# Attention inputs in smaller transfers: keys and queries in two pieces, values in four, each waiting for the piece four places ahead

## What is computed

```python
# q, k, v: (2, 8, 768, 64); tokens 2*768 = 1536, features 8*64 = 512
k_sum = k.reshape(B, H, 24, 32, D).max(axis=3)      # one maximum per block of 32 keys
v_sum = v.reshape(B, H, 24, 32, D).mean(axis=3)
scores_l = scale * q @ k.T, kept where |i - j| < 16  # banded
scores_s = scale * q @ k_sum.T + log(32)
a = softmax over [scores_l, scores_s];  attn = a @ [v, v_sum]
x = attn as (1536, 512)
x = relu(x @ w_in) ** 2 @ w_out                      # d_ff = 2048
h = x @ w_in2;  g = P(h) / Q(h);  out = g @ w_out2   # P cubic, Q of |h| and h*h
```

## Time and profile before

| what | value |
|---|---|
| median of three runs | 594.11 us (592.52 to 595.53) |
| the profiled execution's own time | 595.49 us |
| its span | 593.6 us |
| granted TensorE clock | full speed in all slices |
| matmul busy | 584.5 us, 98% |
| VectorE, ScalarE, GpSimd busy | 409.4, 290.6, 154.8 us |
| moved by DMA | 31.42 MB, most of it in the first 75 us and in the stretches in which weights are loaded |
| attention | 0 to about 72 us |

### The profile page before, as it was taken

One profiled execution on the slowest core, in us unless ns is written; L12 is line 12 of the kernel. 1 busy time (PEld: TensorE's weight loads), 2 busy tenths in 40 slices (PEclk: granted clock), 3 DMA queues, 4 the chain that ended last, 5 costly groups with the idle time before them and its releaser, 6 DMA issues.

```text
span 593.6 us, 10634 instructions
## 1 busy us (share of the span) xinstructions
PE 584.5 (98%) x3770; PEld 478.9 (81%) x3770; DVE 409.4 (69%) x791; ACT 290.6 (49%) x613; POOL 154.8 (26%) x159
## 2 busy tenths in 40 slices
PE   8999999999999999999999999999999999999997
PEld 5777788888888888888888888888888888888885
DVE  5888797663433233456666788888888888888885
ACT  5989511101301110311011887777777777867775
POOL 3768920000300000400000354353342212222221
PEclk9999999999999999999999999999999999999999
DMA  7886470000000000033223200000100000100001
GB/s 243 229 251 181 150 272 0 1 0 1 1 0 0 0 0 0 0 108 106 80 97 107 71 1 1 0 0 1 71 0 0 0 0 0 72 0 1 0 1 71
DMA packets 11618, 31.42 MB, mean 53 GB/s; under 512 B 1600, under 2 KB 2112, under 8 KB 11584
## 3 DMA queue, kind: packets, MB, share of 16 engines
q1 hardware_dynamic: 11296, 30.68, 15.9%
q10 hardware_dynamic: 288, 0.26, 0.1%
HBM read 27.79 MB, written 3.15 MB: 52 GB/s over the span
## 4 chain that ended last, share of the span: by engine, by line
PE 96%; ACT 2%; issue 1%; DVE 1%; POOL 0%; DVEq 0%
PE bank L565 44%; PE bank L633 22%; PE bank L650 22%; PE bank L551 2%; PE bank L535 2%; PE bank L501 1%; ACT prob L715 1%; PE bank L521 1%; PE bank L510 1%; PE bank L590 1%; PE bank L528 0%; DVE prob L934 0%; POOL prob L385 0%; DVE ksum L919 0%; DVE hlo L1079 0%
## 5 line engine op out<-in xcount | busy, mean ns | idle before, releaser
L565 PE MATMUL bank<-xhi,whi 128*128 (+1 forms) x384 | 149.9, 390 | 0.0
L565 PE MATMUL bank<-xhi,wlo 128*128 (+1 forms) x384 | 149.4, 389 | 0.0
L565 PE MATMUL bank<-xlo,whi 128*128 (+1 forms) x384 | 149.4, 389 | 0.0
L732 ACT ACTIVATE hsq<-bank 128x512 f32<-128x512 f32 x48 | 28.8, 600 | 213.2 <-PE bank L565 213.1
L443 POOL TENSOR_TENSOR denom<-denom,habs 128x512 f32<-128x512 f32 (+1 forms) x49 | 66.0, 1348 | 246.1 <-ACT denom L820 246.1
L565 PEld LDWEIGHTS bank<-xhi,wlo 128*128 128x128 f32 x384 | 72.1, 188 | 15.0
L565 PEld LDWEIGHTS bank<-xhi,whi 128*128 128x128 f32 x384 | 72.1, 188 | 14.9
L565 PEld LDWEIGHTS bank<-xlo,whi 128*128 128x128 f32 x384 | 72.0, 188 | 14.8
L650 PE MATMUL bank<-whi,hhi 128*128 128x512 f32 x192 | 75.0, 390 | 0.6 <-DVE hlo L1079 0.6
L1079 DVE TENSOR_TENSOR hlo<-ratio,hhi 128x512 fp32r<-128x512 f32 (+1 forms) x49 | 51.1, 1042 | 34.7 <-ACT hhi L803 34.6
L650 PE MATMUL bank<-wlo,hhi 128*128 128x512 f32 x192 | 74.7, 389 | 0.0
(11 more groups left out here) (80 smaller groups left out, 888.1 us busy)
## 6 DMA issues: line engine op xcount, KB each, us to landing
wraw<-w SPq DMA_DIRECT2D x29, 512.0 KB, 3.4
vwin<-vw SPq DMA_DIRECT2D x16, 288.0 KB, 4.0
out<-osb SPq DMA_DIRECT2D x12, 256.0 KB, 2.1
kraw<-kT SPq DMA_DIRECT2D x7, 384.0 KB, 4.9
q<-qT SPq DMA_DIRECT2D x7, 384.0 KB, 5.0
wraw<-w SPq DMA_DIRECT2D x6, 256.0 KB, 5.0
kraw<-kT SPq DMA_DIRECT2D x2, 128.0 KB, 2.8
q<-qT SPq DMA_DIRECT2D x1, 256.0 KB, 3.7
```

Of the source, the lines that this page charges most:

```text
L565: last = mm(hps[j % 2][:, :], W[a][:, j, kt * P:(kt + 1) * P], X[b][:, kt, bass.ds(CH * c, CH)], start=kt == 0 and i == 0, stop=kt == KT - ...
L732: a.activation(hsq[:, i, :], hps[i][:, :], ACT.Relu).then_inc(h_free, 1)
```

## The change

Keys and queries of a pair-batch n of 1 and more go in two transfers each (768 columns as 2 by 384, 192 KB each), values in four (12 windows as 4 by 3, 144 KB each, for n = 0 too). Each piece has a semaphore of its own. Before it is issued, each piece waits for the landing of the piece four places ahead in the order k, k, q, q, v, v, v, v: keys i for values i of n - 1, queries i for values 2 + i of n - 1, values i for keys i or queries i - 2 of n. The waits that protect buffers stay. TensorE and VectorE wait for each semaphore in turn at the places where they waited for one.

```diff
-    q_in = [sem(f"q_in{r}") for r in range(RING)]
+    q_in = [[sem(f"q_in{r}_{i}") for i in range(2)] for r in range(RING)]
-    k_in = [sem(f"k_in{r}") for r in range(RING)]
-    vw_in = [sem(f"vw_in{r}") for r in range(V_RING)]
+    k_in = [[sem(f"k_in{r}_{i}") for i in range(2)] for r in range(RING)]
+    vw_in = [[sem(f"vw_in{r}_{i}") for i in range(4)] for r in range(V_RING)]
...
         def load_k(n):
             if n >= RING:
                 sp.wait_ge(s_done, GPB * (n - RING + 1) + 1)
-            if n == 1:
-                sp.wait_ge(q_first[0], 16)
-            else:
-                sp.wait_ge(*q_landed(n - 1))
-            sp.dma_start(kraw[n % RING][:, BAND:BAND + S], kT[n]).then_inc(k_in[n % RING], 16)
+            for i in range(2):
+                sp.wait_ge(*vwin_landed(n - 1, i))
+                sp.dma_start(kraw[n % RING][:, BAND + S // 2 * i:BAND + S // 2 * (i + 1)],
+                             kT[n][:, S // 2 * i:S // 2 * (i + 1)]).then_inc(k_in[n % RING][i], 16)
...
         def load_q(n):
             if n >= RING:
                 sp.wait_ge(s_done, GPB * (n - RING + 1) + 2)
-            sp.dma_start(q[n % RING][:, :], qT[n]).then_inc(q_in[n % RING], 16)
+            for i in range(2):
+                sp.wait_ge(*vwin_landed(n - 1, 2 + i))
+                sp.dma_start(q[n % RING][:, S // 2 * i:S // 2 * (i + 1)],
+                             qT[n][:, S // 2 * i:S // 2 * (i + 1)]).then_inc(q_in[n % RING][i], 16)
...
-            if n > 0:
-                sp.wait_ge(*vwin_landed(n - 1))
-            for i, half in enumerate((slice(0, NW // 2), slice(NW // 2, NW))):
-                if n > 0 and i == 1:
-                    sp.wait_ge(*k_landed(n))
-                sp.dma_start(vwin[n % V_RING][0:KW, half, :], vw[n][:, half, :]).then_inc(vw_in[n % V_RING], 16)
+            for i in range(4):
+                if n > 0:
+                    sp.wait_ge(*(q_landed(n, i - 2) if i >= 2 else k_landed(n, i)))
+                part = slice(NW // 4 * i, NW // 4 * (i + 1))
+                sp.dma_start(vwin[n % V_RING][0:KW, part, :], vw[n][:, part, :]).then_inc(vw_in[n % V_RING][i], 16)
...
                 if n > 0:
-                    pe.wait_ge(q_in[r], 16 * (n // RING + (r > 0)))
+                    for i in range(2):
+                        pe.wait_ge(*q_landed(n, i))
...
-                    pe.wait_ge(k_in[r], 16 * (n // RING + (r > 0)))
+                    for i in range(2):
+                        pe.wait_ge(*k_landed(n, i))
...
-            pe.wait_ge(vw_in[n % V_RING], 32 * (n // V_RING + 1))
+            for i in range(4):
+                pe.wait_ge(*vwin_landed(n, i))
...
-                dve.wait_ge(k_in[r], 16 * (n // RING + (r > 0)))
+                for i in range(2):
+                    dve.wait_ge(*k_landed(n, i))
```

More of the change, by code:

```diff
@@ L236, in landing, with k_landed, q_landed, vwin_landed @@
         return (index - EARLY) % LAND, k + (index - EARLY) // LAND
[L238 to L248, removed]
+    def k_landed(n, i):
+        return k_in[n % RING][i], 16 * (n // RING + (n % RING > 0))
+    def q_landed(n, i):
+        return q_in[n % RING][i], 16 * (n // RING + (n % RING > 0))
+    def vwin_landed(n, i):
+        return vw_in[n % V_RING][i], 16 * (n // V_RING + 1)
     block = nc.Block()
```

## The result

The changed kernel takes 597.88 us (median of five runs, 597.36 to 598.08) against 595.26 us for the kernel before (median of five, 592.52 to 596.98). The ratio is 1.0061, with a 95% interval of 1.0041 to 1.0081: slower by 0.6%, some 3.6 us. The two medians alone lie 2.6 us apart, close to the lower end of that interval. The profiled execution has a span of 595.8 us, 2.2 us above the one of before; but that one lay 1.4 us above the median of the first three runs. So the two traces, read against each other, can account for 2.2 to 2.3 us and not for 3.6.

A forecast was written before the change was run, and what follows sets the result against it. TensorE was taken as the bound, its matmuls covering 584.5 of 593.6 us. Waits 0, issues 0 and landings 0 summed to 0, applied to the median of 594.11 us: 594.0 us, range 591.5 to 597.0.

The forecast's parts named there:

- T: Loads at the loop's start: time from a piece's issue to landing with four pieces under way, taken as 2.7 us.
- the one chain into which it was put: Values 0 to keys 3, one T per landing: keys 3 in at 20.2 us, inside 1.8 us of slack, cost 0.
- The straight line through the three sizes: Upper estimate of landing time from 128, 288 and 384 KB transfers: 2.9 us at 144 KB, 3.3 at 192, 3.1 average.
- The test of the pace: Load rounds in the attention: 2T = 5.4 us against the 7.0 us TensorE needs, so loads stay ahead.
- Rival B: Landings at the start slower than before, keys 3 stall TensorE before scores(8): 595.1 us at T = 3.1; chance 0.20.
- its second sign: Sign toward slower landings: a DMA by name among TensorE's waits, the alternative to a VectorE wait near 22 us.
- B's formula: TensorE loses time before scores(8) once keys 3, in at 3.97 + 6T, pass 19.77 + 1.8 us.
- The waits on TensorE: 38 more satisfied waits in scores and summaries: cost 0, upper bound 0.4 us.
- The 30 more issues on SyncE: 12 us more work on SyncE, hidden in its waiting time: cost 0, or 0.8 us once if uncovered.
- Rival A: TensorE's "issue" stalls (1.1 and 1.2 us, no visible cause) before 75 us vanish: 591.8 us, at best 590.9; chance 0.13.
- Rival C: 38 new instructions shift TensorE's code cuts; a 1.1 us stall comes or goes: 593.0 to 595.2 us; chance 0.12.

The follow-up runs named there:

- The count of places: The change with each piece waiting for the one three, five, six or eight places ahead, not four: 1.0195, 1.0020, 1.0009, 1.0006 against the kernel before.
- the kernel with the gap filled: The changed kernel plus seven 128-column matmuls where TensorE had waited 1.78 us for queries of pair-batch 2: 1.0070 against the kernel before, 599.4 us.
- the 38 waits: The kernel before with its loads untouched and 38 more satisfied waits on TensorE: 1.0010, 594.37 us beside 594.35.
- the bare stop: The kernel before, with TensorE also waiting for the keys of pair-batch 3 ahead of the scores of group 6: 1.0048, 597.69 us.
- the late start with six: The change with the first four pieces of pair-batch 1 held back as before, later ones waiting six places ahead: 0.9997 against the kernel before, 594.07 us.
- keys and queries 1 freed: The change, but keys and queries of pair-batch 1 do not wait for values of 0: 1.0072 against the kernel before, 598.52 us.

## Why the prediction was wrong, point by point

**Where the time is.** Right: nothing after 75 us moved, and the first feed-forward matmul came 2.30 us later. I had said under 1 us. Keys 1 were issued at 6.18 us, near the 6.3 forecast; VectorE's wait for keys 4 shrank from 0.82 to 0.45 us (now called "issue") and did not go. Wrong: that loads can only act where TensorE stands still. Of the 2.3 us, 1.6 us is busy time, nearly all of it (1.47 us) matmuls at the lower clock behind the stop.

**The step that failed is T, the time to landing, and the one chain into which it was put.** I took T = 2.7 us from a row of 128 KB at the start. Measured were 3.2, 2.9 and 3.9 us for values, keys and queries, weighted by their 32, 14 and 14 pieces 3.3 us. The straight line through the three sizes, which I had as the upper bound, gave 3.1 us and was nearer. I argued it down because less would be queued. The count of places shows how far that holds: with three places, values landed in 2.5 us, but keys and queries still took 3.3. The estimate of 2.4 us from the Trainium skill ("DMA: Bandwidth & Descriptors", "Anatomy of one DMA") was lower still; that section is on transfers issued by GpSimd, these are issued by SyncE, and the trace's 3.3 us decides.

The chain was wrong too. I followed only the keys, over VectorE. The chain that ended last runs through the queries: from the values issued at 4.30 us to the landing of queries 2 at 19.92 us it has four landings of 3.32 + 4.41 + 2.09 + 5.38 = 15.2 us, 3.8 us each, where my T gives 10.8. The scores of group 6 wait for these queries directly. At T = 2.7 they would have landed at 15.1 us and had 2.8 us to spare against 17.87; even at the mean of 3.3 they would have been in time, at 17.5. It took the long landings of single pieces, which no mean shows: the two halves of queries 2 took 5.5 us in the median. They also held back the keys of pair-batch 3. These were issued at 20.34 us, behind the last quarter of values 2, which had to wait for queries 2, and SyncE runs its program in order. That (23.75 - 3.97)/6 = 3.30 us agrees with the mean is therefore partly luck.

**The test of the pace was too weak.** I compared 2T with the 7.0 us that TensorE needs, found it smaller, and held the loads safe. With 4 pieces of 168 KB, 0.69 MB, under way and T = 3.3 us the rate is 209 GB/s, as the profile shows (207 from 14 to 28 us). A round then takes 6.6 us, and with the waiting between landing and issue 6.9 on average, single rounds 6.1 to 7.8: against 7.0 us that holds the pace but makes up little. Loads have to be faster than their user to win the lead that the start lacks.

**Rival B had the cause right, and the path wrong.** I gave it 0.20. Its threshold, T = 2.93, was passed, and its second sign came, a DMA by name among TensorE's waits. But TensorE never stopped for its path, keys 3 to block maxima to `masked(6)`: the scores of group 8 start at 26.38 us back to back with the work before them, as the stop for queries 2 and the slow stretch had already made TensorE later than keys 3 would have. (In the kernel with the gap filled these scores begin 25.61 - 24.33 = 1.28 us behind the block maxima; 23.75 + 1.28 = 25.0 us here, an estimate.) By B's formula T = 3.3 costs 3.97 + 19.8 - 21.57 = 2.2 us. That this is also the difference of the spans is luck: what made it up is the late keys of pair-batch 6, issued 6.3 us later than before where keys 3 had been 4.4 us late, less the "issue" stops of before that are gone. B's own path shows where the stop is filled with matmuls: the scores of group 8 then wait 0.59 us for VectorE, and with two whole transfers under way 1.55 us.

**The waits on TensorE**, 0 with 0.4 as a bound: nothing against it, though 1.0010 has an interval that is too wide (up to 2 us) to bear out a bound of 0.4 us. **The 30 more issues on SyncE**: with the waits of before, split transfers cost 0.14%, 0.8 us, where I had 0. What of that is issuing and what shorter rows was not tried.

**Rival A** (the "issue" stops shrink when less is queued): its sign came as well, no "issue" line of over 1 us, and in the traces this gave back 2.3 us, less than the late loads took. The 0.6 us that the list still calls "issue" are before the first scores of pair-batch 1, at 12.51 us, right behind the landing of their queries at 12.42 us in the chain; most likely they are a load too, and so is the 1.0 us of the kernel with three places (landing at 12.82, scores at 12.91 us). The traces of all five kernels with three or four pieces or two whole transfers under way have no other such stop. Of the nine with more under way six have one or more of 0.2 to 1.3 us, and three (eight places, the 38 waits, the bare stop) have none. There is one trace for each kernel, so whether the stops belong to a kernel or to an execution, and whether less queueing ends them, stays open. That such a stop counts is seen from the kernel with 38 more waits: its profiled execution has neither and a span of 590.9 us, 2.7 us below that of before, while its median is that of before. **Rival C** (they move with the code) stays open in the same way.

No version beat the kernel before: six and eight places, and the late start with six, agree with it within their intervals.

## What to carry to other kernels

When transfers are cut up and each waits for one some places ahead, count the bytes under way first: divide them by the time to landing that a row with that much queued shows, and compare with the rate that is needed while the lead is still being built, not with the mean need. If it is near, add places; here four were too few, six enough and eight no better. The number of transfers is not without effect: the same bytes in two whole ones moved 199 GB/s where four pieces moved 215. Follow the chain of every tile to whoever waits for it, also of those that nobody waits for yet; here it was the queries, not the keys. A load that is late by little can cost TensorE twice, by the stop and by the lower clock behind it; whether that reaches the end depends on the loads behind it.

## What the runs showed of the hardware that was not expected

- The time to landing went by the bytes under way more than by the size. With 0.69 MB under way 144 KB and 288 KB of values both took 3.2 us, 192 KB and 384 KB of queries 3.9 and 3.8 us, of keys 2.9 and 3.7 us. The same 144 KB took 2.5 us with three pieces under way and 4.5 us with six.
- The queries were slowest or level with the slowest with three to five places (3.3, 3.9, 4.0 us), though the keys have the same shape (3.3, 2.9, 3.0 us) and are issued just ahead of them. Why was not tried.
- Stops of TensorE of 1.7 to 1.9 us in the attention were followed by a granted clock of 0.50 to 0.71 for some 4 us (the change, the bare stop) or of 0.50 from 20 to 28 us (keys and queries 1 freed); with matmuls in most of the gap and 1.06 us idle, the clock stayed at 1.00. But with three places a stop of 2.39 us, up to 24.97 us, left it at 1.00 too, as did those of 1.1 and 1.2 us in the kernel before, so the length of the stop alone does not decide. What does was not tried.
